# Attention with windows, then two feed-forward blocks: where SyncE issues its loads, and how VectorE and ScalarE share a pair of head groups

## The reference, cut to what matters

```python
B, H, S, D = 2, 8, 768, 64        # q, k, v; n_global = 8, n_local = 96
scores = q @ k.T / sqrt(D)
keep = is_global | is_local       # first 8 keys, and the 96 keys up to the query
scores += -slopes[h] * dist       # dist is n_local for global keys that aren't local
scores = where(keep, scores, -1e9) - max
a = exp(scores);  a = a / (sum(a) + 1e-9)
x = (a @ v), heads side by side   # 768 x 512 for each of 2 batches
# block 1: token mixing by U (768 x 32) and V, then a feed-forward 512 -> 2048 -> 512
u = x + (x.T @ U @ V).T;   y = u + relu(u @ w_ch1) @ w_ch2
# block 2: gated, with a mixing over tokens
h = relu(y @ w_in);  u2, v2 = halves of h;  v_n = normalised v2
out = (u2 * (w_spatial @ v_n + b_spatial)) @ w_out
```

## Time and profile before

| | |
|---|---|
| three runs | 521.18, 521.78 and 521.9 us; median 521.78 |
| the profiled execution | 521.44 us, its span 519.3 us, mean granted clock 0.984 |
| busy: PE, DVE, ACT, POOL | 491.6, 318.5, 219.5, 250.3 us |
| weigh of quad 23 starts | 116.83 us after the span's start |

### The profile page before, as it was taken

How to read it: one execution, slowest core, us unless ns; L and a number is a source line. 1 busy time by engine, 2 the same in 40 slices (tenths; PEclk the granted TensorE clock), 3 DMA queues, 4 the chain that set the end, 5 groups by cost and what they waited for, 6 DMA issues and landing times.

```text
span 519.3 us, 7912 instructions
## 1 busy us (share of the span) xinstructions
PE 491.6 (95%) x2756; PEld 410.6 (79%) x2756; DVE 318.5 (61%) x753; ACT 219.5 (42%) x496; POOL 250.3 (48%) x221
## 2 busy tenths in 40 slices
PE   8786878879999999999999999999999999999997
PEld 7565756668778888888888888888888888898986
DVE  5776767851214945556466565465878889879500
ACT  6676557852322454334234223131544236533121
POOL 6587345643333577574556662550697300870000
PEclk9799889989999999999999999999999999999999
DMA  8344333223222242012222202210011300000022
GB/s 237 128 133 152 112 113 113 77 71 114 103 82 81 83 154 90 22 61 81 82 81 81 82 0 83 81 32 30 2 60 62 112 1 1 1 0 37 25 82 101
DMA packets 19016, 39.47 MB, mean 76 GB/s; under 512 B 3744, under 2 KB 7072, under 8 KB 18976
## 3 DMA queue, kind: packets, MB, share of 16 engines
q1 hardware_dynamic: 16960, 35.55, 20.8%
q10 hardware_dynamic: 2016, 3.41, 1.8%
HBM read 35.75 MB, written 3.19 MB: 75 GB/s over the span
## 4 chain that ended last, share of the span: by engine, by line
PE 64%; DVE 10%; DMA 8%; ACT 5%; POOL 4%; SPq 4%; issue 3%; DVEq 2%; ACTq 0%
PE bank L1830 14%; PE bank L1764 8%; PE bank L1688 8%; PE bank L1912 8%; PE bank L1859 7%; PE bank L1852 7%; PE bank L1555 6%; DMA inv_scratch<-inv_T 6%; ACT prob L1218 3%; SPq L413 2%; POOL sp_op L627 1%; PE bank L1613 1%; DVE prob L797 1%; DVEq L1047 1%; DVE newton L1059 1%
## 5 line engine op out<-in xcount | busy, mean ns | idle before, releaser
L572 POOL TENSOR_TENSOR w_slot<-stage,w_slot 128x1024 fp32r<-128x1024 f32 x30 | 73.3, 2452 | 68.8 <-ACT w_slot L1288 68.8
L979 DVE TENSOR_TENSOR uT<-bank,uT 128x512 f32<-128x512 f32 x68 | 45.8, 689 | 25.2 <-PE bank L1859 23.2
L1218 ACT ACTIVATE prob<-prob,row_min 128x256 f32<-128x256 f32 (+1 forms) x96 | 45.9, 480 | 23.9 <-DVE row_min L797 23.8
L1830 PE MATMUL bank<-u_op,s_slot 128*128 128x512 f32 x192 | 47.6, 389 | 0.0
L1764 PE MATMUL bank<-hid,w_slot 128*128 128x512 f32 x192 | 46.9, 393 | 0.0
L1688 PE MATMUL bank<-u_split,w_slot 128*128 128x512 f32 x192 | 46.4, 391 | 0.0
L1852 PE MATMUL bank<-hid,w_slot 128*128 128x512 f32 x192 | 46.1, 389 | 0.0
L1859 PE MATMUL bank<-hid,w_slot 128*128 128x512 f32 x192 | 46.1, 389 | 0.0
L1017 DVE TENSOR_TENSOR part<-part,bank 128x512 f32<-128x512 f32 x40 | 27.4, 685 | 26.8 <-PE bank L1830 26.4
L1764 PEld LDWEIGHTS bank<-hid,w_slot 128*128 128x128 f32 x192 | 35.7, 188 | 8.2 <-issue 0.9
L1830 PEld LDWEIGHTS bank<-u_op,s_slot 128*128 128x128 f32 x192 | 36.0, 188 | 7.5
(11 more groups left out here) (151 smaller groups left out, 974.8 us busy)
## 6 DMA issues: line engine op xcount, KB each, us to landing
stage<-in_w_ch SPq DMA_DIRECT2D x32, 512.0 KB, 3.3
qk_raw<-in_qk SPq DMA_DIRECT2D x23, 256.0 KB, 3.3
v_all<-in_v SPq DMA_DIRECT2D x12, 256.0 KB, 3.0
inv_rows<-inv_scratch SPq DMA_DIRECT2D x48, 64.0 KB, 2.6
out_dram<-o_stage ACTq DMA_DIRECT2D x11, 256.0 KB, 2.0
stage<-in_w_spT SPq DMA_DIRECT2D x6, 384.0 KB, 3.0
stage<-in_w_in SPq DMA_DIRECT2D x4, 512.0 KB, 3.7
stage<-in_w_out SPq DMA_DIRECT2D x2, 512.0 KB, 3.8
```

Source lines behind the costliest of these rows:

```text
L572: nc.gpsimd.tensor_tensor(dst[:, LO, :], stage[n % 2][:, 0:w], dst[:, HI, :].bitcast(F32), ALU.subtract).then_inc(w_lo, 1)
L979: vec.tensor_tensor(y, y_bank(e)[:], y, ALU.add).then_inc(y_sum, 1)
L1218: last = sc.activation(prob[r][:, e, 0:w], prob[r][:, e, 0:w], ACT.Exp, bias=row_min[:, k:k + 1], scale=-1.0, accum_out=row_sum[:, q:q + 1])
L1830: last = mm(seven_bank[held][:], lhs, u_op[op][:, m, k, :], start=not more and k == 0 and p == 0, stop=k == 1 and p == 2, skip_group_check ...
```

## The change

SyncE now issues the loads between the store of the inverse and its spread. q and k are loaded by quad and not by tile (`load_quad`), and the first two weight loads are cut into eight pieces of 32 rows, one for each of the quads 4 to 11. ScalarE copies pair 0 of the transposed probabilities and VectorE pair 1 (before, the other way round). The minima and the exponentials of a quad are two halves with the copies and the scaling between them. ScalarE adds the 1e-9 (`add_eps`), VectorE did before. The two early roundings of weights move from s = 13 and 19 to s = 11 and 12.

In the new order VectorE's step s (s >= 1) is score_bias(s+2, 0), invert(s+1), turn_inverse(s+1), scale_x(s-1), score_bias(s+2, 1), take_probT(s+1), and ScalarE's is exps(s+2, 0), take_probT(s+1), take_x(s-1), exps(s+2, 1), add_eps(s+2). TensorE's order is the same.

```diff
--- before.py
+++ after.py
@@ -276,6 +276,10 @@
                  + [("sp", s) for s in range(NT)] + [("out", 0), ("out", 1)])
         STAGES = len(LOADS)
 
+        def staged(n):
+
+            return 16 * (n // 2 + 4)
+
         def load_no(*what):
             return LOADS.index(what)
 
@@ -379,16 +383,20 @@
         def _(sp):
             def load_qk(t):
                 r = t % 3
-                if t >= 3:
-
-                    if t == 3:
-                        sp.wait_ge(qk0_lo, 2)
-                    else:
-                        sp.wait_ge(qk_lo, 2 * (t - 3))
                 for hq in range(1 if t == 0 else 0, 2):
 
                     c = slice(2 * hq, 2 * hq + 2)
                     sp.dma_start(qk_raw[r][:, c, :, :], qk[t, :, c, :, :]).then_inc(qk_in[r][hq], 16)
+
+            def load_quad(g):
+
+                t, hq = divmod(g, 2)
+                c = slice(2 * hq, 2 * hq + 2)
+                if t == 3:
+                    sp.wait_ge(qk0_lo, hq + 1)
+                else:
+                    sp.wait_ge(qk_lo, g - 7)
+                sp.dma_start(qk_raw[t % 3][:, c, :, :], qk[t, :, c, :, :]).then_inc(qk_in[t % 3][hq], 16)
 
             def load_v(t):
                 b, i = divmod(t, NT)
@@ -418,8 +426,17 @@
                 for g in range(REP):
                     sp.dma_start(V_raw[g * R:(g + 1) * R, :], V).then_inc(V_in, 16)
 
+            def load_piece(n, c):
+
+                rows = slice(32 * c, 32 * c + 32)
+                sp.dma_start(stage[n][rows, :], w_ch[LOADS[n][1]][rows, :]).then_inc(stage_in[n], 16)
+
             def load_stage(n):
                 kind, k = LOADS[n]
+                if n < EARLY:
+                    for c in range(4):
+                        load_piece(n, c)
+                    return
                 if n >= 2:
                     sp.wait_ge(w_lo, n - 1)
                     kind2, m = LOADS[n - 2]
@@ -441,23 +458,23 @@
                 load_v(0)
                 load_v(1)
                 load_V()
-                load_qk(3)
+                load_quad(6)
+                load_quad(7)
                 load_v(2)
                 load_v(3)
                 for g in range(QUADS):
+                    store_inverse(g)
+                    if g + 8 < QUADS:
+                        load_quad(g + 8)
+                    if g in (1, 3):
+                        load_v((g + 7) // 2)
+                    if 4 <= g < 12:
+                        load_piece((g - 4) // 4, g % 4)
                     if g == 11:
                         load_v(NT)
-                    store_inverse(g)
-                    spread_inverse(g)
-                    if g % 2 == 0 and g // 2 + 4 < TILES:
-                        load_qk(g // 2 + 4)
-                    if g in (1, 3):
-                        load_v((g + 7) // 2)
                     if g % 2 and g >= 11 and (g + 3) // 2 < TILES:
                         load_v((g + 3) // 2)
-                    if g == 6:
-                        load_stage(0)
-                        load_stage(1)
+                    spread_inverse(g)
             with sp.Else():
                 load_V()
                 for n in range(EARLY):
@@ -596,8 +613,8 @@
                 def dst(name):
                     return s_raw[i % 2][:, SUMS[name], :]
 
-                pool.wait_ge(stage_in[(n - 1) % 2], 16 * ((n - 1) // 2 + 1))
-                pool.wait_ge(stage_in[n % 2], 16 * (n // 2 + 1))
+                pool.wait_ge(stage_in[(n - 1) % 2], staged(n - 1))
+                pool.wait_ge(stage_in[n % 2], staged(n))
                 if i == 0:
                     pool.wait_ge(pv_done, QUADS)
                 elif i == 1:
@@ -802,19 +819,17 @@
 
             def take_probT(g):
                 w = 2 * P * blocks(g // 2)
-                dve.wait_ge(turned, 2 * g + 1)
+                if g < 2:
+
+                    dve.wait_ge(turned, 2 * g + 1)
+                    vec.tensor_copy(probT[2 * g][:, 0:w], pt_bank[0][:, 0:w]).then_inc(probT_a, 1)
+                dve.wait_ge(turned, 2 * g + 2)
                 if g >= 2:
                     dve.wait_ge(pv_done, g - 1)
-                vec.tensor_copy(probT[2 * g % 4][:, 0:w], pt_bank[0][:, 0:w]).then_inc(probT_d, 1)
-                if g < 2:
-
-                    dve.wait_ge(turned, 2 * g + 2)
-                    vec.tensor_copy(probT[2 * g + 1][:, 0:w], pt_bank[1][:, 0:w]).then_inc(probT_a, 1)
+                vec.tensor_copy(probT[(2 * g + 1) % 4][:, 0:w], pt_bank[1][:, 0:w]).then_inc(probT_d, 1)
 
             def invert(g):
                 q = slice(g % 4 * 4, g % 4 * 4 + 4)
-                dve.wait_ge(expd, 2 * g + 2)
-                vec.tensor_scalar(row_one[:, q], row_sum[:, q], 1e-9, None, ALU.add).then_inc(sum_eps, 1)
                 dve.wait_ge(sum_eps, g + 1)
                 if g == 0:
                     dve.wait_ge(inv_set, 2)
@@ -909,19 +924,15 @@
                 for r in range(2):
                     vec.memset(row_inv[r][:], 0.0).then_inc(inv_set, 1)
                 for s in range(-2, QUADS + 1):
-                    if 0 <= s < QUADS and s != 2:
-                        take_probT(s)
+                    if s + 2 < QUADS:
+                        score_bias(s + 2, 0)
+                        if s < 1:
+                            score_bias(s + 2, 1)
                     if 0 <= s + 1 < QUADS:
+                        if s < 1:
+                            take_probT(s + 1)
                         invert(s + 1)
-                    if 0 <= s + 1 < QUADS:
                         turn_inverse(s + 1)
-                    if s in (0, 1, 12):
-                        score_bias(s + 2, 0)
-                        if s == 1:
-                            take_probT(2)
-                        score_bias(s + 2, 1)
-                    elif 0 <= s + 2 < QUADS:
-                        score_bias(s + 2)
                     if s >= 1:
                         scale_x(s - 1)
                     if s == 15:
@@ -929,6 +940,11 @@
                     for j in range(FIRST):
                         if s == MIX_AT[j]:
                             sum_u(j)
+                    if s >= 1:
+                        if s + 2 < QUADS:
+                            score_bias(s + 2, 1)
+                        if s + 1 < QUADS:
+                            take_probT(s + 1)
             with dve.Else():
                 dve.sem_inc(w_o, 1)
                 dve.wait_ge(w_tables, 2)
@@ -1206,11 +1222,11 @@
                     sc.activation(bias[:, h, :], dist[:], ACT.Copy, scale=-(2.0 ** -(h + 1)) / SCALE
                                   ).then_inc(bias_set, 1)
 
-            def exps(g, half=None):
+            def exps(g, half):
                 w = P * blocks(g // 2)
                 if g >= 4:
                     act.wait_ge(sum_eps, g - 3)
-                for m in range(2) if half is None else (half,):
+                for m in (half,):
                     r = (2 * g + m) % 4
                     act.wait_ge(biased, 2 * g + m + 1)
                     for e in range(2):
@@ -1221,10 +1237,16 @@
 
             def take_probT(g):
                 w = 2 * P * blocks(g // 2)
-                act.wait_ge(turned, 2 * g + 2)
-                if g >= 2:
-                    act.wait_ge(pv_done, g - 1)
-                sc.activation(probT[(2 * g + 1) % 4][:, 0:w], pt_bank[1][:, 0:w], ACT.Copy).then_inc(probT_a, 1)
+                act.wait_ge(turned, 2 * g + 1)
+                act.wait_ge(pv_done, g - 1)
+                sc.activation(probT[2 * g % 4][:, 0:w], pt_bank[0][:, 0:w], ACT.Copy).then_inc(probT_a, 1)
+
+            def add_eps(g):
+                q = slice(g % 4 * 4, g % 4 * 4 + 4)
+                act.wait_ge(expd, 2 * g + 2)
+                if g >= 4:
+                    act.wait_ge(inv_ok, g - 3)
+                sc.activation(row_one[:, q], row_sum[:, q], ACT.Copy, bias=1e-9).then_inc(sum_eps, 1)
 
             def take_x(g):
 
@@ -1271,7 +1293,7 @@
             def split_stage(n):
                 dst, w = stage_dst(n)
                 kind, k = LOADS[n]
-                act.wait_ge(stage_in[n % 2], 16 * (n // 2 + 1))
+                act.wait_ge(stage_in[n % 2], staged(n))
                 if kind == "w":
                     if 3 <= k < 6:
                         act.wait_ge(pv_done, QUADS)
@@ -1294,30 +1316,31 @@
 
             near = windowed(act)
             with act.If(near):
-                for s in range(-2, QUADS):
-                    if s >= 3:
-                        take_probT(s)
-                    if s == 13:
-                        split_stage(0)
+                for s in range(-2, QUADS - 1):
+                    g = s + 2
+                    if s == -2:
+                        set_bias(0)
+                    if g < QUADS:
+                        exps(g, 0)
+                        if s < 1 or s == GATHER:
+                            exps(g, 1)
+                            add_eps(g)
                     if s == GATHER:
```

(27 more changed lines are left out.)

## The result

The kernel after takes 504.02 us (median of four runs, 502.93 to 504.92), the kernel before 521.84 beside it. The ratio is 0.9642 with a 95% interval of 0.9588 to 0.9696: 3.6% faster. The profiled execution took 504.92 us, its span is 503.0.

What follows compares the result with a forecast made beforehand. SyncE's chain of store, spread and loads was taken to bound the attention part. Quad 23's weighing: 24.4 + 20 x 3.40 + 4.6 - 1.2 + 3.0 = 98.8 against 116.83, 18.0 us saved, so 503.8 us; range 498.5 to 512.

Steps and rivals of the forecast that it cites:

- SyncE is the bound, and moving the loads into the flight frees it: SyncE's store, spread and loads: period about 4.6 us before, 3.02 (3.53 at the other end) with loads inside the store's flight.
- The signs: Expected in the trace: store to spread 1.8 to 2.0, stores 3.3 to 3.5 apart, no landing over 3 after quad 2.
- The old order would be the next bound: ScalarE: x copy ahead of the second exponentials removes most of the 7.9 us that weighing waited for it.
- A step of 3.40: Steady loop of quads: 3.32 us a step by count, taken as 3.40 for varying hand-overs, against 4.47 before.
- S+3.25: VectorE's probT copy in the steady loop ends 3.25 us after S, the end of the scores two steps ahead.
- the case that I gave 0.13: Rival for the steady loop: hand-overs hide completely, TensorE bounds steps at 3.18 us, total 496.4 (in part, 500); chance 0.13.
- Quad 3 at 24.4: Start-up: weighing of quad 3 at about 24.4 us instead of 27.36, 3.0 us saved (between 1 and 4).
- Extras of 6.4 in the 20 steps: Quads 3 to 23: 4.6 us for gather, fold and mixes, less 1.2 for half-sized quads, plus 3.0 of ripple.
- Pieces instead of whole weight loads: SyncE's stage loads, one piece per step in quads 4 to 11: removes the 4.98 us landing, priced inside the per-step account.
- the second rival: Landings stay late, spreads directly behind loads: 3.6 to 3.8 us a step, total 506.4 to 510.4; chance 0.20.

Runs made afterwards that it cites:

- the list alone: Kernel before with only SyncE's new list (loads between store and spread, by quad, weights in pieces), engines' order as before: 512.98 us, ratio to before 0.9831.
- the run with the epsilon on it: Kernel after with the 1e-9 added on VectorE again, behind a wait for the quad's last exponential: 505.18 us, ratio to before 0.9679.
- the run with the copy first: Kernel after with GpSimd's last two low parts of u moved behind its copy of V rows for quad 23: 502.94 us, ratio to before 0.9627.

## Why the prediction was right

The time was right to 0.2 us (503.8 forecast, 504.02 measured), its steps less so. That it came so close is luck: three errors of 2.1 to 4.6 us cancel, and the execution from which the steps are read was the slowest of the four, 0.9 above their median.

- *SyncE is the bound, and moving the loads into the flight frees it*: right for the new order, half right for the kernel before. Store to spread is 1.64 to 2.08 for quads 1 to 7, SyncE's periods 3.03 to 3.24 with one exception (4.87), near my 3.02, and with the loads behind the spreads again TensorE waits for the scaling in step after step. But the reading of before went from one mean, 4.47 a step, to one bound, SyncE's 4.6. The run with the list alone shows that up to quad 8 ScalarE's x copy held the steps (4.04 on average in both) and that SyncE's lag came due in single stops, 4.3 us of it at quad 9. The account came out right because it priced the new order by its own count, and not by taking the list's gain off the old steps.
- *The signs*: stores were to be 3.3 to 3.5 apart and no landing over 3 behind quad 2. The stores are closer, and there are such landings: quad 8's store in 3.11, quad 11's to its spread 3.66, single spreads up to 4.0. Two stores of before are also missing from the counts of the earlier trace rows: quad 1's, behind loads, took 3.06, and quad 22's, with none ahead, 2.59. The sum doesn't rest on them.
- *The old order would be the next bound*, implied by the x copy's wait in the earlier trace rows: right; the list alone gives 512.98.
- *A step of 3.40*: too high. Of the six steps from quad 3 to quad 9 five take 3.17 or 3.18 and one 3.25; TensorE's own is 3.18. The count put VectorE's copy at S+3.25 and a hand-over of 0.2 behind it. Measured, from the scores' end near 32.86 to 35.91, it is S+3.05, and where VectorE is last (the run with the epsilon on it) the weighing follows 0.04 behind the copy. So the case that I gave 0.13 (TensorE is the bound) is the right one for the steady loop. Over 20 steps that is 4.6 us.
- *Quad 3 at 24.4*: 26.51. The scaling of quad 0 came at 18.91 as worked out (18.5), but I counted what follows at full speed. TensorE had idled 3.71, and four groups behind it took 0.67, 0.88, 0.88 and 0.31 more than usual, 2.7 in all. The trace of before had the same pattern at 53 to 57, and I used it there and not here. Part of the 2.1 us is scatter: four variants with the same start weigh quad 3 at 24.69, 25.24, 25.37 and 26.46.
- *Extras of 6.4 in the 20 steps*: 10.0 (73.36 less 20 x 3.17). Three stops make 4.3 of it together: quad 10 (0.8, a late spread), quad 12 (1.9, four loads in one flight and V behind them; I had priced these at 0.5 to 1.1 of SyncE's time and nothing on TensorE), and quad 23 (1.6, the difference to the run with the copy first: GpSimd's copy stands behind two low parts that wait for ScalarE). The last I had not seen at all: I followed GpSimd's list only for lateness by a step, not for what stands in it behind ScalarE's roundings. The rest is 5.7 against my 6.4.
- Together: +2.1 - 4.6 + 3.6 = +1.1 on the weighing of quad 23: 99.87 against the forecast 98.8.
- *Pieces instead of whole weight loads*: priced inside the account, and the run with whole loads says they are worth nothing in the new order. The 4.98 landing of the earlier trace rows hurt because it stood on SyncE's critical list; in flight it is mostly hidden.
- *Spreads behind loads may land late*, the second rival: true as an event, not as a bound. The median landing is 2.6 in both kernels, but single spreads took 4.0 in after, and 4.55, 4.70 and 4.73 in three variants (quad 13's). The rule of the Trainium skill ("DMA: Bandwidth & Descriptors", section "Queues, rings and completion order") is that the completion increment comes only after every earlier write of that DMA engine. The run with whole weight loads agrees: the last 512 KB load ahead of quad 6's spread landed at 40.38, the spread's two DMAs at 40.34 and 40.90. For quad 13's spreads the rule isn't enough, since the q/k and V loads ahead of them had landed 2.6 to 2.8 us before they did. The next q/k load, issued about 1.2 us behind these spreads, landed 0.6 behind them in all three traces; whether it held them up was not tested.

## What to carry to other kernels

When a queue issues a round trip and also carries bulk loads, put the loads into the flight of the first leg, not behind the last leg: moving the same loads from one place to the other costs 18 us here, of which about a quarter is one V tile that came too late for its own use. Two loads mostly fit into a flight of 1.9 us; with three and four the spread went out up to 4.72 and 3.77 behind its store. Before a queue is called the bound of every step, compare the steps one by one: here the list alone changed none of the first eight. Such a fix and the order of the engines that wait for the round trip have to be changed together, for each alone uncovers the other. A stop of TensorE can cost more than it lasts, since 2.7 us of slow products came on top of the 3.71, so price the next products at the lower clock too, as a risk: stops of 1.49, 2.16, 2.56 and 3.71 us were followed by products at about half speed, stops of 1.41, 2.13 and 2.17 in other traces were not. When one engine's list is reordered, follow the lists of the others to the end of the phase.

## What was not expected of the hardware

- The time of one kernel scatters by 2 to 8 us with nothing changed. Single late landings of small DMAs (up to 4.73 us, median 2.6) are part of it: in two traces one stood ahead of a step of 8.4 and 8.5 us (4.87 in after). They come without loads ahead, too: in two traces a spread near the end, issued when every load before it had landed, took 3.6 and 3.7.
- SyncE's issue of the same load took 0.43 us in the flight of a store and 0.58 directly behind a spread. A weight piece, 0.43 in most steps, took 3.04 once as the third load of a flight. Why is open.
- A store that goes out directly behind loads waits 1.9 to 3.3 us to the spread; with a spread in between mostly 1.64 to 2.1 (in after 19 of quads 1 to 23, the others 2.45, 2.47, 3.13 and 3.66). The loads are not through by then: in after those issued at 31.76 and 32.23 landed at 34.78 and 35.39, and the store at 34.33 still took only 1.97. Why it isn't held up is open.
- An add of four columns on VectorE that starts beside an instruction of GpSimd ends with that one: it took up to 1.56 us instead of 0.17.
